# Startup of a fused attention and gated-dense kernel: task order, a second state buffer, moved neighbour sums and a moved weight copy

## The chip, the cores and the metric

The kernel runs on one core of a Trainium2 chip. The metric is the device time of one execution in microseconds (us), and the number compared is the median of several runs. Five parts of the core matter: TensorE (PE) with its weight loads (PEld), VectorE (DVE), ScalarE (ACT), GpSimd (POOL), and SyncE (SP), which issues all DMAs here. Each has its own queue of instructions and works through it strictly in order; they meet only through semaphores.

## The reference

Three computations follow each other: a linear attention with a decaying state, a gated dense part, and a mixture of four experts.

```python
def _attn_ref(q, k, v, alpha) -> np.ndarray:          # (4, 8, 768, 48) each
    state = np.zeros((B, H, D, D), dtype=np.float32)
    for t in range(S):
        state = alpha[:, :, t, :, None] * state + np.einsum('bhd,bhe->bhde', k[:, :, t], v[:, :, t])
        y[:, :, t] = np.einsum('bhd,bhde->bhe', q[:, :, t], state)

def _moe_ref(x, w_gate, w_val, w_out) -> np.ndarray:  # x: 3072 x 384, d_ff 1536
    gate = 1.0 / (1.0 + np.exp(-(x @ w_gate)))
    return (gate * (x @ w_val) @ w_out).astype(np.float32)

def _moe2_ref(x, domain_probs, w1, w2) -> np.ndarray: # 4 experts of 1024
    for e in range(E):
        out += p[:, e:e + 1] * (np.maximum(x @ w1[e], 0.0) @ w2[e])
```

## The kernel before

**Tiling.** The 768 positions of each of the 4 batches are cut into chunks of 128, so there are 24 attention *steps*, numbered 0 to 23 here. Three steps make one tile of 384 tokens for the gated dense part, which for each of 12 slices of d_ff runs a `gate` group, a `value` group (9 matmuls each into one bank) and an `out` group (9 matmuls). The experts come after all 8 tiles and are not touched here.

**One attention step.** The pairs inside a chunk are covered by six *levels* (`LVL`): at each, ACT spreads the needed columns of q into `QX` (L958), PE multiplies them with k (L695, L698), and the result goes into the matrix `AT`, by DVE under a mask for levels 0 to 2 (L1235) and by ACT for levels 3 to 5 (L929, L935). DVE multiplies k and q by the decays after each level (L1177); the next level's spread waits for that. Then come `TRK` (PE turns k, ACT copies it to `Kn`), `STATE` (PE makes the chunk's addition to the state from `Kn` and `V`, DVE scales the old state `ST` and adds it: L1249, L1255), `YOUT` (PE multiplies q with the state of the step before, L714, and `V` with `AT`, L718; DVE adds the part of the nearest neighbours and writes `ynat`, L1243) and `TRX` (PE turns `ynat`, ACT and DVE write its high and low half, `xT0h` and `xT0l`).

**Neighbour sums.** The terms of a position with itself and with the position before it are made apart: POOL multiplies rows (`near_products`, L1468 to L1471, three instructions), DVE sums them over each head (`near_sums`, L1204, into `near`), POOL multiplies with V and adds (`near_terms`, L1478 twice and L1484, into `y_near`). `near` and `y_near` have two buffers each.

**The first three steps.** They have no dense work to stand beside. They run in the order of the list `FIRST`, which all engines follow. The tasks use three banks of PSUM in turn, so that each task waits for the reader of the task three places before. At its end `first_part` does gate and value of slice 0 for the tokens of steps 0 and 1 (256 columns), and then for those of step 2 (128 columns). Then the tile loop starts: the remaining groups of tile 0, with the tasks of steps 3, 4 and 5 in slots between them. `prepare(0, 3)` on DVE (L1186, L1188, L1192) reads the k, q and decays of step 3, and stands in DVE's queue ahead of the first product of gate and value (`hid`, L1270).

**Weights.** `w_gate`, `w_val` and `w_out` arrive in three pieces each and are split into a high half, a rounded copy (`WGh` and so on), and a low half, the difference (`WGl` and so on). For the first three pieces `low_raw1(n)` does that on POOL: a cast (L1520) and a subtraction (L1522); of piece 0 alone the high half is made by ACT (`high_raw1(0)`, after level 2 of step 0). Piece 1 is the first of `w_val`, piece 2 the first of `w_out`. The semaphore `raw_split` counts the subtractions.

**The queue of SP.** There are six buffers for raw pieces, and piece n + 6 is loaded only when `raw_split` has reached n + 1. In the order of the queue:

```python
for n in range(len(pieces)):
    if n == len(pieces) - 1:
        load_step(0, STEPS_T)      # k, q and decays of step 3
        load_rows(0, STEPS_T)
    load_raw(n)                    # n >= 6 waits for raw_split >= n - 5
```

So piece 7 waits for the low half of piece 1, and what follows in the queue waits with it: first the `KQ` load of step 3 (which itself waits for step 1's state, y and neighbour terms), then `row` and `V` of step 3, then piece 8.

## Time and profile before

| | us |
|---|---|
| median of 3 runs | 1394.03 (1392.42 to 1394.73) |
| time of the profiled execution | 1391.0 |
| its span, first to last instruction | 1389.2 |
| PE busy | 1361.9 (98%) |
| POOL busy | 963.8 (69%) |
| DVE busy | 852.0 (61%) |
| ACT busy | 738.2 (53%) |
| TensorE clock granted | 1.0 over the whole span |

The page divides the span in 40 slices of about 35 us. PE is at nine tenths or more in nearly all of them; the first slice has 5 and the second 8 to 9. What is said below of the change concerns the first two slices. Times in the timeline are from the span's start; "x8" is a count of instructions merged into one row, and a bracket gives the idle time before and what ended it.

### The profile page before, as it was taken

How to read it: one execution, taken by the hardware profiler on the slowest of the kernel's cores; microseconds unless marked ns; L12 is line 12 of the kernel's file. 1: busy time of each engine (PE TensorE's matmuls, PEld its weight loads, DVE VectorE, ACT ScalarE, POOL GpSimd, SP SyncE). 2: the span in 40 equal slices, each digit the busy share in tenths (PEclk: the TensorE clock that was granted, in tenths of full speed). 3: DMA queues.
4: the chain of work that ended last, by engine and by line, in shares of the span. 5: the costliest groups of instructions: out<-in, count | busy, mean ns of one | idle time of the engine just before them, and what ended most of it. 6: DMA issues, size and time to landing. Idle time of an engine off the chain costs nothing.

```text
span 1389.2 us, 27651 instructions
## 1 busy us (share of the span) xinstructions
PE 1361.9 (98%) x10026; PEld 1261.6 (91%) x10026; DVE 852.0 (61%) x1335; ACT 738.2 (53%) x1467; POOL 963.8 (69%) x942
## 2 busy tenths in 40 slices
PE   5989999999999999999999999999999999999998
PEld 4989999999999999998999999999999999999998
DVE  7786555546464556343666666666766666666666
ACT  6664545445454455345555555555755555555552
POOL 6685545445445447477889898987897777777772
PEclk9999999999999999999999999999999999999999
DMA  9422221312121312002010101010121010101001
GB/s 326 122 76 89 89 75 55 109 56 84 62 75 55 109 55 88 13 1 69 24 46 24 46 24 45 23 46 23 46 92 46 24 46 24 45 23 45 23 12 68
DMA packets 42403, 83.37 MB, mean 60 GB/s; under 512 B 5824, under 2 KB 31168, under 8 KB 42304
## 3 DMA queue, kind: packets, MB, share of 16 engines
q1 hardware_dynamic: 42304, 82.01, 18.4%
q8 instruction: 67, 1.10, 0.3%
q14 instruction: 32, 0.26, 0.1%
HBM read 77.28 MB, written 4.72 MB: 59 GB/s over the span
## 4 chain that ended last, share of the span: by engine, by line
PE 95%; DVE 3%; ACT 1%; issue 1%; DMA 1%; POOL 0%; POOLq 0%; SPq 0%; ACTq 0%; DVEq 0%
PE PS L863 29%; PE PS L852 24%; PE PS L747 22%; PE PS L757 11%; PE PS L695 4%; PE PS L718 2%; PE PS L714 1%; PE PS L698 1%; DVE KQ L1177 1%; PE PS L703 1%; PE PS L726 1%; DMA KQ<-in_qka 1%; PE PS L731 0%; DVE AT L1235 0%; ACT QX L958 0%
## 5 line engine op out<-in xcount | busy, mean ns | idle before, releaser
L1417 DVE SCALAR_TENSOR_TENSOR acc<-PS,prob,acc 128x384 f32<-128x384 f32 x360 | 221.8, 616 | 209.6 <-PE PS L863 209.6
L958 ACT ACTIVATE QX<-KQ 48x256 f32<-48x256 f32 x288 | 120.8, 420 | 130.1 <-DVE KQ L1177 107.6
L1079 ACT ACTIVATE mixed<-PS 128x512 f32<-128x512 f32 x192 | 112.6, 589 | 89.8 <-PE PS L852 89.0
L1177 DVE TENSOR_TENSOR KQ<-KQ,TOT 112x512 f32<-112x512 f32 (+1 forms) x126 | 109.8, 894 | 43.6 <-PE PS L695 25.4
L1270 DVE TENSOR_TENSOR hid<-PS,hid 128x384 f32<-128x384 f32 x96 | 53.5, 558 | 128.2 <-PE PS L747 113.9
L1107 ACT ACTIVATE mixed<-mixed 128x512 f32<-128x512 f32 x192 | 118.4, 617 | 0.0
L1501 POOL TENSOR_TENSOR hs1l<-hid,hs1h 128x384 fp32r<-128x384 f32 x48 | 53.1, 1106 | 87.2 <-ACT hs1h L977 87.2
L1501 POOL TENSOR_TENSOR hs0l<-hid,hs0h 128x384 fp32r<-128x384 f32 x48 | 54.7, 1140 | 76.9 <-ACT hs0h L977 76.8
L695 PE MATMUL PS<-QX,KQ 112*64 112x64 f32 x1920 | 81.9, 237 | 20.4 <-ACT QX L958 19.7
L695 PEld LDWEIGHTS PS<-QX,KQ 112*64 112x64 f32 x1920 | 71.3, 148 | 32.8 <-issue 16.7
L1106 ACT ACTIVATE H_1h<-mixed 128x512 fp32r<-128x512 f32 x32 | 20.3, 634 | 129.9 <-DVE mixed L1391 129.9
L973 ACT ACTIVATE hid<-PS 128x384 f32<-128x384 f32 x96 | 47.2, 492 | 60.3 <-PE PS L747 57.4
L1461 POOL TENSOR_TENSOR TOT<-TOT 112x128 f32<-112x128 f32 (+2 forms) x126 | 43.2, 343 | 49.4 <-DVE TOT L1186 41.1
L1468 POOL TENSOR_TENSOR row<-row 128x384 f32<-128x384 f32 x24 | 24.2, 1007 | 63.7 <-DMA V<-in_v 63.7
L1235 DVE COPY_PREDICATED AT<-mask,PS 128x512 f32<-128x512 int32 x72 | 66.2, 919 | 0.5
L1629 POOL TENSOR_TENSOR H_0l<-mixed,H_0h 128x512 fp32r<-128x512 f32 x32 | 41.6, 1301 | 28.7 <-ACT mixed L1107 28.7
L1629 POOL TENSOR_TENSOR H_4l<-mixed,H_4h 128x512 fp32r<-128x512 f32 x32 | 41.5, 1297 | 24.5 <-ACT mixed L1107 24.5
L977 ACT ACTIVATE hs1h<-hid 128x384 fp32r<-128x384 f32 x48 | 25.2, 526 | 55.0 <-DVE hid L1270 55.0
L1629 POOL TENSOR_TENSOR H_5l<-mixed,H_5h 128x512 fp32r<-128x512 f32 x32 | 41.6, 1299 | 15.4 <-ACT mixed L1107 15.4
L1617 POOL TENSOR_TENSOR W_1l<-w_sum,W_1h 128x1408 fp32r<-128x1408 f32 x16 | 52.0, 3251 | 0.0
L1617 POOL TENSOR_TENSOR W_0l<-w_sum,W_0h 128x1408 fp32r<-128x1408 f32 x16 | 52.0, 3250 | 0.0
L747 PE MATMUL PS<-xT1h,WGh 128*128 128x384 f32 x144 | 50.1, 348 | 0.5 <-DVE xT1l L1263 0.5
(536 smaller groups left out, 4950.3 us busy)
## 6 DMA issues: line engine op xcount, KB each, us to landing
row<-in_rows SPq DMA_DIRECT2D x24, 768.0 KB, 4.4
KQ<-in_qka SPq DMA_DIRECT2D x24, 672.0 KB, 4.8
rawA<-in_w SPq DMA_DIRECT2D x32, 384.0 KB, 3.1
rawB<-in_w SPq DMA_DIRECT2D x32, 384.0 KB, 3.3
V<-in_v SPq DMA_DIRECT2D x24, 384.0 KB, 4.8
out_y<-acc SPq DMA_DIRECT2D x24, 192.0 KB, 2.2
raw<-in_w_gate SPq DMA_DIRECT2D x3, 768.0 KB, 13.9
raw<-in_w_val SPq DMA_DIRECT2D x3, 768.0 KB, 13.5
```

The source lines that it names most:

```text
L695: mm = pe.matmul(dst[mine, :, right], KQ[p][0:R, 1, a, mine], cols[:, :, right], start=True, stop=True)
L747: mm = pe.matmul(PS[:, bank, 0:T1], W[w][:, n, f * P:(f + 1) * P], xT[p][x][:, n, :], start=(n == 0 and (w, x) == SPLITS[0]), stop=(n == K ...
L757: mm = pe.matmul(PS[:, out_bank0 + n, 0:T1], WO[w][:, f, n * P:(n + 1) * P], hs[f % 2][x][:], start=(f == 0 and (w, x) == SPLITS[0]), stop ...
L852: mm = pe.matmul(PS[:, hidden_banks[HIDDEN[g]], :], W1[u % 2][w][:, WEIGHT[g], :], x_block(q, g)[x][:], start=n == 0 and g not in CONTINUE ...
L863: mm = pe.matmul(PS[:, result_banks[at % 4], 0:DM], h[x][:, t * P:(t + 1) * P], W2[u % 2][w][:, m, :], start=(m == 0 and (w, x) == SPLITS[ ...
L958: done = nc.scalar.activation(QX[p][rows, :, g, :].rearrange("d a (n t) -> d a n t", t=2 << level), right, ACT.Copy)
L1079: nc.scalar.activation(mixed[:, COPIED[g], :], PS[:, hidden_banks[HIDDEN[g]], :], ACT.Copy).then_inc(copied, 1)
L1107: nc.scalar.activation(mixed[:, part, :], mixed[:, part, :], ACT.Relu).then_inc(rh_ready, 1)
L1177: dve.tensor_tensor(x, x, y, ALU.mult).then_inc(kq_ready[p], 1)
L1417: dve.scalar_tensor_tensor(out=to, in0=result, scalar=weight, in1=to, op0=ALU.mult, op1=ALU.add).then_inc(acc_ready, 1)
L1501: nc.gpsimd.tensor_tensor(hs[f % 2][1][:], hid[f % 2][:], hs[f % 2][0][:].bitcast(F32), ALU.subtract).then_inc(hl_ready, 1)
L1629: nc.gpsimd.tensor_tensor(low[:], mixed[:, part, :], high[:].bitcast(F32), ALU.subtract).then_inc(rl_ready, 1)
```

## The change

- Order: in `FIRST`, `TRK` of step 1 comes ahead of `YOUT` of step 0, `STATE` of step 1 ahead of `YOUT` of step 1, and `YOUT` of step 2 between the `TRX` of steps 0 and 1. The gate part over steps 0 and 1 now follows `TRX` of step 2.
- State: a second buffer `ST1` holds the state after step 1. It lies over the last part of the low half of `w_val`, which is written much later.
- Neighbour sums: `near` gets a third buffer; the three `near_sums` on DVE move to after (level 5, step 0), (level 3, step 2) and (level 5, step 1). On POOL `near_products` of step 2 moves ahead of all `near_terms`, and `near_terms` of step 2 ahead of `low_raw1(1)`.
- Weight copy: the high half of piece 0 is made by POOL, and no more by ACT.

```diff
     if n == LEVELS:
-        FIRST += [(STATE, 0, 0), (YOUT, 0, 0), (TRK, 1, 0)]
-FIRST += [(YOUT, 1, 0), (STATE, 1, 0), (TRX, 0, 0), (TRX, 1, 0), (YOUT, 2, 0), (TRK, 2, 0), (TRX, 2, 0), (STATE, 2, 0)]
+        FIRST += [(STATE, 0, 0), (TRK, 1, 0), (YOUT, 0, 0)]
+FIRST += [(STATE, 1, 0), (YOUT, 1, 0), (TRX, 0, 0), (YOUT, 2, 0), (TRX, 1, 0), (TRK, 2, 0), (TRX, 2, 0), (STATE, 2, 0)]
...
+        ST1 = nc.alloc_sbuf_tensor_at("ST1", [P, PAIRS, 2 * D], F32, offset=top[0] - PAIRS * 2 * D * 4)
...
+        def state_of(i, sc):
+            return ST1 if is_first(i, sc) and sc == 1 else ST
...
-                if t == (YOUT, STEPS_T - 1, 0):
+                if t == (TRX, STEPS_T - 1, 0):
                     first_part("gate", 0, STEPS_T - 1)
-                if t == (TRX, STEPS_T - 1, 0):
                     first_part("value", 0, STEPS_T - 1)
...
-            high_after = {(LVL, 0, 2): 0}
...
-                if t in high_after:
-                    high_raw1(high_after[t])
...
-                        dve.tensor_tensor(ST[0:R], ST[0:R], tot_of(i, sc, C)[0:R].to_broadcast([R, PAIRS, 2 * D]),
+                        to = state_of(i, sc)
+                        dve.tensor_tensor(to[0:R], state_of(i, sc - 1)[0:R], tot_of(i, sc, C)[0:R].to_broadcast([R, PAIRS, 2 * D]),
...
-            sums_after = {(LVL, 0, 3): 0, (LVL, 0, 4): 1, (LVL, 1, 5): 2}
+            sums_after = {(LVL, 0, 5): 0, (LVL, 2, 3): 1, (LVL, 1, 5): 2}
...
-                if n == 0:
-                    pool.wait_ge(weight_high, 1)
-                else:
-                    pool.wait_ge(raw1_in[n], 16)
-                    nc.gpsimd.tensor_copy(high, raw_piece(n)).then_inc(own_high, 1)
-                    pool.wait_ge(own_high, n)
+                pool.wait_ge(raw1_in[n], 16)
+                nc.gpsimd.tensor_copy(high, raw_piece(n)).then_inc(own_high, 1)
+                pool.wait_ge(own_high, n + 1)
...
             low_raw1(0)
+            near_products(0, 2)
             near_terms(0, 0)
             near_terms(0, 1)
-            near_products(0, 2)
+            near_terms(0, 2)
             low_raw1(1)
-            near_terms(0, 2)
             low_raw1(2)
```

The queue of POOL between the row products of step 1 and the decays of step 3, before. `row_113` and `row_114` are the rows of steps 1 and 2, `raw_53` the raw pieces, `V_63`, `V_74`, `V_134` the V of steps 0, 1, 2:

```order
L1522 TENSOR_TENSOR WGl<-raw_53,WGh 128x3x512
L1478 TENSOR_TENSOR row<-V_63,near_81 128x384 x2
L1484 TENSOR_TENSOR y_near_83<-row 128x384
L1478 TENSOR_TENSOR row_113<-V_74,near_82 128x384 x2
L1484 TENSOR_TENSOR y_near_84<-row_113 128x384
L1468 TENSOR_TENSOR row_114<-row_114 128x384
L1469 TENSOR_TENSOR row_114<-row_114 128x384
L1471 TENSOR_TENSOR row_114<-row_114 128x384
L1520 CAST WVh<-raw_53 128x3x512
L1522 TENSOR_TENSOR WVl<-raw_53,WVh 128x3x512
L1478 TENSOR_TENSOR row_114<-V_134,near_81 128x384 x2
L1484 TENSOR_TENSOR y_near_83<-row_114 128x384
```

The same stretch in the changed kernel (its lines are 1 to 7 higher; `row_115`, `row_116`, `V_136` are now the names of steps 1 and 2, and `y_near_84` that of the first buffer):

```order
L1521 CAST WGh<-raw_53 128x3x512
L1523 TENSOR_TENSOR WGl<-raw_53,WGh 128x3x512
L1472 TENSOR_TENSOR row_116<-row_116 128x384
L1473 TENSOR_TENSOR row_116<-row_116 128x384
L1475 TENSOR_TENSOR row_116<-row_116 128x384
L1482 TENSOR_TENSOR row<-V_63,near_81 128x384 x2
L1488 TENSOR_TENSOR y_near_84<-row 128x384
L1482 TENSOR_TENSOR row_115<-V_74,near_82 128x384 x2
L1488 TENSOR_TENSOR y_near_85<-row_115 128x384
L1482 TENSOR_TENSOR row_116<-V_136,near_83 128x384 x2
L1488 TENSOR_TENSOR y_near_84<-row_116 128x384
L1521 CAST WVh<-raw_53 128x3x512
```

A cast is added at the head, and the split of piece 1 (`WVh`, `WVl`) now stands behind all three `y_near`, the last of which writes the buffer that step 0 used.

On PE, from the first `STATE` to the state matmuls of step 1, before (`AT_64` is step 0's, `KQ_65` step 1's, `KQ_125` step 2's):

```order
L726 MATMUL PS<-V_63,Kn 48x48 x8
L718 MATMUL PS<-V_63,AT_64 64x48 x16
L703 MATMUL PS<-ident,KQ_65 128x112 x4
L698 MATMUL PS<-QX_126,KQ_125 64x128 x4
L714 MATMUL PS<-ST,KQ_65 64x96 x2
```

and in the changed kernel (`KQ_127` is step 2's):

```order
L733 MATMUL PS<-V_63,Kn 48x48 x8
L710 MATMUL PS<-ident,KQ_65 128x112 x4
L725 MATMUL PS<-V_63,AT_64 64x48 x16
L705 MATMUL PS<-QX_128,KQ_127 64x128 x4
L733 MATMUL PS<-V_74,Kn 48x48 x8
L721 MATMUL PS<-ST,KQ_65 64x96 x2
```

The transpose of step 1's k moved up by one place and its `STATE` matmuls (`V_74,Kn`) moved ahead of its `YOUT`.

## Rows read from the trace of the kernel before

**Rows 1.** The page, the chain that ended last, by engine.

```profile
PE 95%; DVE 3%; ACT 1%; issue 1%; DMA 1%; POOL 0%; POOLq 0%; SPq 0%; ACTq 0%; DVEq 0%
```

**Rows 2.** Busy time by stretch: PE, PEld, DVE, ACT, POOL, then clock, DMA share, GB/s.

```profile
50.00:66.00 16.00, 16.00 (x135) 14.69 (x136) 12.43 (x18) 10.56 (x18) 9.19 (x12) 1.00 0.34 77
66.00:81.00 15.00, 12.59 (x123) 11.23 (x120) 15.00 (x17) 11.52 (x22) 11.59 (x14) 1.00 0.20 67
```

**Rows 3.** The chain of waits in order of time, two pieces of the start.

```profile
24.85 0.42 ACT QX L958
...
34.79 1.12 PE PS L695 x16
```

**Rows 4.** Timeline of ACT: start, duration, line, tiles.

```profile
18.73 1.49 ACT L1048 ACTIVATE WGh<-raw 128x1536 fp32r<-128x1536 f32 x1 [0.71 <-DMA raw<-in_w_gate]
20.12 1.69 ACT L958 ACTIVATE QX<-KQ 48x256 f32<-48x256 f32 x4
```

**Rows 5.** Timeline of DVE, from 21 to 52 us.

```profile
21.94 0.95 DVE L1204 TENSOR_REDUCE near<-row 128x16 f32<-128x768 f32 x1
22.80 0.69 DVE L1177 TENSOR_TENSOR KQ<-KQ,PS 112x512 f32<-112x512 f32 x1
...
38.37 0.56 DVE L1243 TENSOR_TENSOR ynat<-PS,y_near 128x384 f32<-128x384 f32 x1 [0.94 <-PE PS L718]
...
41.56 0.54 DVE L1249 TENSOR_TENSOR ST<-ST,PS 112x384 f32<-112x384 f32 x1
...
49.84 0.43 DVE L1186 TENSOR_TENSOR TOT<-KQ 112x256 f32<-112x256 f32 x1
...
51.44 0.56 DVE L1270 TENSOR_TENSOR hid<-PS,hid 128x384 f32<-128x384 f32 x1
```

**Rows 6.** Timeline of PE, from 36 to 53 us.

```profile
36.32 1.94 PE L718 MATMUL PS<-V,AT 128*64 128x48 f32 x32
38.19 0.60 PE L703 MATMUL PS<-ident,KQ 112*128 112x112 f32 x4
...
43.11 0.39 PE L714 MATMUL PS<-ST,KQ 112*64 112x96 f32 x4 [0.81 <-DVE ST L1255]
...
44.84 0.38 PE L780 MATMUL PS<-xT0h,WGh 128*128 128x256 f32 x1
...
52.09 0.40 PE L747 MATMUL PS<-xT0h,WVh 128*128 128x384 f32 x1
```

**Rows 7.** Timeline of POOL, from 18 to 41 us.

```profile
18.60 1.01 POOL L1471 TENSOR_TENSOR row<-row 128x384 f32<-128x384 f32 x1
...
29.89 1.00 POOL L1468 TENSOR_TENSOR row<-row 128x384 f32<-128x384 f32 x1
...
32.74 1.47 POOL L1520 CAST WVh<-raw 128x1536 fp32r<-128x1536 f32 x1
34.29 3.45 POOL L1522 TENSOR_TENSOR WVl<-raw,WVh 128x1536 fp32r<-128x1536 f32 x1
37.70 1.62 POOL L1478 TENSOR_TENSOR row<-V,near 128x384 f32<-128x384 f32 x2
39.40 1.00 POOL L1484 TENSOR_TENSOR y_near<-row 128x384 f32<-128x384 f32 x1
40.34 1.47 POOL L1520 CAST WOh<-raw 128x1536 fp32r<-128x1536 f32 x1
```

**Rows 8.** Timeline of SP: two issues.

```profile
37.77 0.37 SPq L612 DMA_DIRECT2D raw<-in_w_val  x1
41.41 0.33 SPq L592 DMA_DIRECT2D KQ<-in_qka  x1
```

**Rows 9.** SP's waits: who, for whom, total, times, longest.

```profile
SPq L612 <- POOL WVl L1522: 13.3, 1, 13.3
```

**Rows 10.** DMA issues by narrow window: KB, us to landing (issued 37.77, 41.41, 48.65).

```profile
raw<-in_w_val SPq DMA_DIRECT2D x1, 768.0 KB, 4.4
...
KQ<-in_qka SPq DMA_DIRECT2D x1, 672.0 KB, 4.6
...
KQ<-in_qka SPq DMA_DIRECT2D x1, 672.0 KB, 9.8
```

**Rows 11.** The first two KQ loads: waits of DVE, and the transfer's piece in the chain.

```profile
5.82 0.43 DVE L1186 TENSOR_TENSOR PS<-KQ 112x256 f32<-112x256 f32 x1 [1.66 <-DMA KQ<-in_qka]
...
8.41 0.43 DVE L1186 TENSOR_TENSOR PS<-KQ 112x256 f32<-112x256 f32 x1 [1.23 <-DMA KQ<-in_qka]
...
1.21 7.17 DMA KQ<-in_qka
```

More of the change, by code:

```diff
@@ L324, in attention_moe_program @@
         row = sb("row", [P, 4, DM])
-        near = [sb(f"near{p}", [P, 2, H]) for p in range(2)]
+        near = [sb(f"near{p}", [P, 2, H]) for p in range(3)]
         y_near = [sb(f"y_near{p}", [P, DM]) for p in range(2)]
@@ L507, in ynat_of, with near_of @@
             return ynat1 if is_first(i, sc) and sc == 1 else ynat
+        def near_of(i, sc):
+            return near[buffer_of(i, sc)]
+        def state_of(i, sc):
+            return ST1 if is_first(i, sc) and sc == 1 else ST
         def row_of(i, sc):
@@ L713, in task @@
                         for mine in sides if chunk else ():
-                            pe.matmul(bank[mine, a * 2 * D:(a + 1) * 2 * D], KQ[p][0:R, 0, a, mine], ST[0:R, a, :],
+                            pe.matmul(bank[mine, a * 2 * D:(a + 1) * 2 * D], KQ[p][0:R, 0, a, mine], state_of(i, sc - 1)[0:R, a, :],
                                       start=True, stop=False, skip_group_check=True)
@@ L1203, in near_sums @@
                 wait_apart(dve, products_ready, per_step(i, sc, 1, 1), sums_seen)
-                dve.tensor_reduce(near[sc % 2][:], row_of(i, sc)[:, 2:4, :].rearrange("p w (h d) -> p w h d", d=D), AX.X,
+                dve.tensor_reduce(near_of(i, sc)[:], row_of(i, sc)[:, 2:4, :].rearrange("p w (h d) -> p w h d", d=D), AX.X,
                                   ALU.add).then_inc(near_ready, 1)
@@ L1254, in task @@
                         if chunk:
-                            done = dve.tensor_tensor(ST[rows, :, mine], ST[rows, :, mine], new[rows, :, mine], ALU.add)
+                            done = dve.tensor_tensor(to[rows, :, mine], to[rows, :, mine], new[rows, :, mine], ALU.add)
                         else:
@@ L1283, in low_part1 @@
                 high, low = weight_parts(n)
-                dve.wait_ge(weight_high, n - 1)
+                dve.wait_ge(weight_high, n - 2)
                 done = dve.tensor_tensor(low[:, k], raw_piece(n)[:, k], high[:, k].bitcast(F32), ALU.subtract)
@@ L1479, in near_terms @@
                                             V[p][:, w].rearrange("p (h d) -> p h d", d=D),
-                                            near[sc % 2][:, w].unsqueeze(2).to_broadcast([P, H, D]), ALU.mult).then_inc(near_part, 1)
+                                            near_of(i, sc)[:, w].unsqueeze(2).to_broadcast([P, H, D]), ALU.mult).then_inc(near_part, 1)
                 pool.wait_ge(near_part, per_step(i, sc, 2, 2))
@@ L1526, in low_part1 @@
                 high, low = weight_parts(n)
-                pool.wait_ge(weight_high, n - 1)
+                pool.wait_ge(weight_high, n - 2)
                 done = nc.gpsimd.tensor_tensor(low[:, k], raw_piece(n)[:, k], high[:, k].bitcast(F32), ALU.subtract)
```

## Prediction

> **What bounds the kernel now.** I first read the page's chain of the work that ended last. PE is 95% of it [rows 1], so the kernel is a long row of PE work, and a change of the first 50 us counts only by how much earlier or later PE enters that row. The busy times by stretch show where it begins: PE is busy for all 16.00 us from 50 to 66, and from 66 to 81 for 12.59 of 15.00, while DVE is then busy for 15.00 [rows 2]. The work of that second stretch follows from the first (DVE's next product of gate and value waits for PE), so I treat what comes behind about 52 us as one rigid block, which moves with its first late piece. Next the chain of the start: from 24.85 it runs through ACT's copies without a gap to 34.79, where PE starts level 4 of step 2 [rows 3]; before 24.85 it is DVE. From 34.79 it alternates between PE and DVE, with one stall of PE, 0.81 us at 43.11, where step 2's YOUT waits for the state [rows 6].
>
> I take the start of the value group of slice 1, at 52.09, as the mark [rows 6]. It waits for the first `hid` of DVE, 51.44 + 0.56 = 52.00 [rows 5]. So PE's own queue and DVE's arrive within 0.1 us of each other: PE alone can gain nothing unless `hid` comes earlier too. This is the point on which I decide.
>
> **The change, part by part.**
>
> *Weight copy and neighbour sums.* ACT loses the copy of piece 0; from its start to the next one's is 20.12 - 18.73 = 1.39 us [rows 4]. DVE loses the first sum at 21.94, which costs 22.80 - 21.94 = 0.86 us there [rows 5], and the second, of the same form, a level later; both go to places where DVE waits for PE. The chain piece at 24.85 is an ACT copy that waits for DVE, so it comes earlier by the smaller of what both give: 0.86, not 1.39 + 0.86. ACT then runs through as before, and level 4 of step 2 starts at 34.79 - 0.86 = 33.93.
>
> *Order and second state.* From 33.93 I lay PE's tasks in the new order with their distances of before: the step 0 state matmuls at 34.8, step 1's k transpose at 35.46, step 0's YOUT at 35.98 (before 36.32), level 5 of step 2 after 1.87 us (38.19 - 36.32 [rows 6]) at 37.85. Then step 1's STATE 0.5 us on, its YOUT at 38.8. DVE's two steps for state 1 take 1.30 us (from 41.56 to 42.86, the point at which the stall ends [rows 5, 6]) and start about 1.5 us behind the level, at 39.3, so the state is there at 40.6. YOUT of step 2 follows at 40.75 without the stall, against 43.11: 2.4 us earlier. `ST1` costs no instruction; it only lets PE still read the old state while DVE writes the new. But gate now stands behind three transposes and needs step 1's x of both halves: TRX of step 1 at 42.5, ACT 0.5, DVE 0.6, each with its hand-over, which gives 44.2, against 44.84. Value follows at 45.4, and as nothing stands between the parts any more, PE's own arrival at the mark is near 50.9, a gain of 1.2 us. With the second sum and the third buffer of `near` nothing else moves: they only make the late sums possible.
>
> *POOL.* Here the bill comes. Its queue is free at 18.60 + 0.96 = 19.56. The added cast takes 1.55 and the subtraction 3.41 (34.29 - 32.74 and 37.70 - 34.29 [rows 7]): 24.5. The row products of step 2 take 2.85 (32.74 - 29.89): 27.4. Then POOL waits for the moved sums: the first ends at about 29.1, the second at 32.2. The terms take 1.70 + 0.94 each (39.40 - 37.70, 40.34 - 39.40 [rows 7]): 31.7, 34.9, and the products of the third end at 36.6. Its last addition writes the buffer that step 0's YOUT reads, so it waits for that: PE 35.98, plus the 2.05 from 36.32 to 38.37, plus 0.56 [rows 5, 6], makes 38.6. Only at 39.6 does the cast of piece 1 start, and its low half is there at 39.6 + 1.55 + 3.45 = 44.6, where it was 37.74. For the value part that is in time (45.4).
>
> *SP.* But SP holds piece 7 until then: it waited 13.3 us for this very subtraction before [rows 9] and issued at 37.77 [rows 8]. Now it issues at 44.6, and the KQ load of step 3, free at 41.41 before, is queued behind and goes at 45.0. Before it needed 4.6 us alone [rows 10] and landed at 46.0, 3.8 us before DVE took it up at 49.84 [rows 5]. That cover is gone.
>
> *When does it land?* No row shows a KQ load issued 0.4 us behind a full piece at this place. Lower bound: the piece ahead costs nothing, 45.0 + 4.6 = 49.6. Upper bound from rows of the same form: the KQ load with most in flight beside it took 9.8 [rows 10], 54.8. Nearest are the first two KQ loads, issued back to back in the same queue: DVE could start with them at 5.82 and 8.41, 2.6 us apart, and the second took 7.17 from its issue [rows 11]. Piece 7 took 4.4 from issue to landing [rows 10], so it lands at 49.0 and KQ 2.6 later at 51.6 (by the 7.17 it would be 52.2). I take 51.6. By the Trainium skill, DMA: Bandwidth & Descriptors, Anatomy of one DMA, a transfer costs about 2.0 us and its bytes at 436 GB/s; its fit is for another issuing path. For KQ alone (688 KB) that gives an estimate of 3.6 us, where the trace has 4.6, and for both loads in flight (1.47 MB) 5.4 us from 44.6, so 50.0 and 0.15 us over before at the mark.
>
> *DVE and the sum.* `prepare(0, 3)` stands ahead of `hid` in DVE's queue; from its start to the end of `hid` it is 52.00 - 49.84 = 2.16 us [rows 5]. With two hand-overs of 0.04: 51.6 + 2.24 = 53.84, later than PE's 50.9, so the gain of the front is lost, and the mark moves by 53.84 - 52.09 = +1.75 us. Behind it: POOL's decays of step 3 wait for the same KQ and end in time (before, the low half of `hid` had 0.5 us to spare, and both shift alike). Row and V of step 3 come later too; POOL needs them for the second low half, which had 1.3 us to spare. The KQ of step 4, issued at 48.65 before, is taken up only after 67 us. I cost these at nothing.
>
> Sum on the profiled execution: 1391.0 + 1.75 = 1392.8 (its span 1389.2 + 1.75 = 1390.9). That execution stood 3.0 us below the median of the runs, so for the median I predict 1394.03 + 1.75 = 1395.8 us.
>
> **The rivals.**
>
> *The load is not slowed by the piece ahead.* For it: SP issues them 0.4 us apart, and a lone load needed 4.6. Against it: the second of the first two loads landed 2.6 us behind the first. It lands at 49.6, the mark is at 51.84, and the time is 1394.03 - 0.25 = 1393.8: no change. (The estimate from the Trainium skill's page above, a landing at 50.0, belongs to this case too: 1394.2.)
>
> *The gain of the front arrives whole.* It needs `hid` by 50.9, so KQ by 48.7, less than 3.7 us after an issue at 45.0, or an issue by 44.1 at 4.6 us. For it: only if step 0's y, and with it POOL's split, comes a good microsecond earlier than I laid it. Time 1394.03 - 1.2 = 1392.8.
>
> *The load falls into a crowd (the slower side).* Row and V of step 3 are issued right behind KQ, and piece 7 ahead of it. If the four share the transfer engines instead of going one after the other, KQ needs as long as the 9.8 us that one took [rows 10]; say 9, landing at 54.0, and the mark is at 56.24, +4.15, 1398.2. It counts as slower from a landing at 52.65 on, which is +2.8. Against it: at 41.41 the same row and V were behind the KQ load, and it took 4.6.
>
> *The change does not do what it says.* If the moved sums made the late term of step 1 late for its YOUT, PE would stall near 40.7. `y_near` of step 1 is ready at 34.9 by my sum, 5.8 us before; I give it no chance of its own.
>
> **How the numbers follow.** The forecast (KQ from 50.5 to 52.6, so +0.7 to +2.8) gets 0.57; no slowing 0.18; the whole gain 0.07; the crowd 0.18. The own range of the forecast is 1394.7 to 1396.8. For 8 in 10, I leave out the end of the whole gain and the outer half of the crowd: 1393.1 to 1398.2. A measurement of this kernel tells about 0.2%, 2.8 us, from no change (its runs before lie 2.3 us apart). Forecast, no slowing and whole gain all lie inside it; the crowd lies outside. Faster 0.03, for what I have not seen and the spread of the medians; same 0.77; slower 0.20.
>
> **What would show it.** On ACT no weight copy near 18.7 and the copy at 24.85 near 24.0. On PE level 4 of step 2 near 33.9, YOUT of step 2 near 40.8 without a stall, the first gate part near 44.2. On POOL the subtraction of `WVl` ending near 44.6; on SP piece 7 right behind it and KQ at 45.0. On DVE an idle time ahead of `prepare(0, 3)` that a DMA of KQ ends, at 51.6, and a stall of PE ahead of the value group of slice 1, released by `hid` at 53.8. I am wrong if DVE does not wait there, or if PE idles elsewhere before 66 us, or if the stretch from 66 to 81 takes another length than before.

## The result, and the profile after

The changed kernel takes 1399.24 us, the median of 7 runs (1397.98 to 1401.02); the kernel before, run beside it, 1394.03 (7 runs). The ratio is 1.0035, with a 95% interval of 1.0024 to 1.0046: 5.2 us slower, where 1.75 were forecast. The time is 3.4 us above the forecast and 1.0 above the upper end of its range. The profiled execution took 1398.29 us, its span is 1396.4.

The chain that ended last, by engine, is nearly the one of [rows 1]:

```profile
PE 94%; DVE 3%; DMA 1%; issue 1%; ACT 1%; POOL 1%; POOLq 0%; SPq 0%; DVEq 0%; ACTq 0%
```

What is new in it stands in one place. This is the chain in order of time (start, duration, what), the answer to [rows 3]:

```profile
35.40 1.12 PE PS L702 x16
...
38.10 1.90 PE PS L725 x32
...
40.10 0.57 DVE ynat L1246
...
40.81 1.00 POOL y_near L1488
41.81 1.42 POOL WVh L1521
...
43.30 3.48 POOL WVl L1523
...
46.80 0.37 SPq L619
...
47.29 7.17 DMA KQ<-in_qka
...
54.48 0.43 DVE TOT L1189
...
56.08 0.57 DVE hid L1274
...
56.69 1.86 PE PS L754 x9
```

The chain runs from PE (step 0's YOUT, 38.10) to DVE, which writes `ynat`; to POOL, whose last neighbour sum may then reuse its buffer and whose split of piece 1 follows; to SP, which had waited for this split; to step 3's KQ load, to DVE's `prepare(0, 3)` and to the mark. Every link is one that the prediction named. Before, the two issues stood at 37.77 and 41.41 [rows 8], and DVE found KQ there at 49.84 [rows 5]. SP's wait for the split, 13.3 us in [rows 9], is now 19.9:

```profile
SPq L619 <- POOL WVl L1523: 19.9, 1, 19.9
```

On PE (start, duration, line; in brackets the idle time before and what ended it), the answer to [rows 6]:

```profile
43.66 0.39 PE L721 MATMUL PS<-ST,KQ 112*64 112x96 f32 x4
...
47.21 0.35 PE L787 MATMUL PS<-xT0h,WGh 128*128 128x256 f32 x1 [0.37 <-DVE xT0l L1267]
...
56.69 0.45 PE L754 MATMUL PS<-xT0h,WVh 128*128 128x384 f32 x1 [2.80 <-DVE hid L1274]
...
99.03 0.69 PE L702 MATMUL PS<-QX,KQ 112*64 112x64 f32 x16 [1.56 <-ACT QX L964]
```

The stall of 0.81 us ahead of step 2's YOUT is gone, as planned, and one of 2.80 us has come at the mark. By stretch (PE, PEld, DVE, ACT, POOL, then clock, DMA share, GB/s), the answer to [rows 2]:

```profile
50.00:66.00 16.00, 13.20 (x107) 12.23 (x104) 10.66 (x16) 7.98 (x14) 9.53 (x12) 1.00 0.79 226
66.00:81.00 15.00, 13.59 (x129) 12.00 (x127) 13.54 (x17) 11.53 (x23) 9.80 (x12) 1.00 0.01 2
...
99.00:104.00 5.00, 4.97 (x32) 4.93 (x33) 2.75 (x4) 3.43 (x8) 4.17 (x6) 0.66 0.00 0
```

PE lost 2.80 us between 50 and 66. The last row was not in the prediction at all: from 99.71, for 3.4 us, the granted clock is 0.50, the lower of TensorE's two levels (1.2 GHz), right behind PE's idle 1.56 us. The profile before has the same idle time, 1.54 us, at that place of the work and no such stretch.

**Where the 7.2 us between the two profiled spans lie.** DVE could start with the second KQ load at 8.41 before [rows 11] and at 9.80 after: 1.39 us of the start that has nothing to do with the change (in two further profiles of the changed kernel it is 8.42 and 9.02, in a second one of the kernel before 9.62). I therefore count the mark from that moment: 52.09 - 8.41 = 43.7 before, 56.69 - 9.80 = 46.9 after, so +3.2. From the mark to the end it is 1337.1 and 1339.7, so +2.6: about 1.5 lie where the clock is low, 1.1 spread over the experts. The fifteen profiles of this study without such a stretch, of whatever kernel, end 1336.6 to 1339.2 behind their mark, so that last 1.1 need not be the change's.

### The profile page after: what moved, and what is told of

The parts are those of the page before. It is cut to its first block, busy times and chain, and to the rows that moved or that the text cites. A ratio compares the mean times of both kernels' runs of the same rounds, so it can differ in the third digit from the quotient of the medians.

```text
span 1396.4 us, 27651 instructions
## 1 busy us (share of the span) xinstructions
PE 1366.4 (98%) x10026; PEld 1268.3 (91%) x10026; DVE 854.8 (61%) x1335; ACT 737.5 (53%) x1466; POOL 966.7 (69%) x943
## 4 chain that ended last, share of the span: by engine, by line
PE 94%; DVE 3%; DMA 1%; issue 1%; ACT 1%; POOL 1%; POOLq 0%; SPq 0%; DVEq 0%; ACTq 0%
PE PS L869 29%; PE PS L858 24%; PE PS L754 22%; PE PS L764 11%; PE PS L702 4%; PE PS L725 1%; DMA KQ<-in_qka 1%; PE PS L721 1%; PE PS L705 1%; DVE KQ L1180 1%; PE PS L710 1%; PE PS L733 0%; PE PS L738 0%; DVE AT L1238 0%; ACT QX L964 0%
## 5 line engine op out<-in xcount | busy, mean ns | idle before, releaser
L1465 POOL TENSOR_TENSOR TOT<-TOT 112x128 f32<-112x128 f32 (+2 forms) x126 | 43.2, 343 | 47.9 <-DVE TOT L1189 39.7
L754 PE MATMUL PS<-xT0h,WVh 128*128 128x384 f32 x141 | 49.7, 352 | 2.8 <-DVE hid L1274 2.8
```

The lines of the kernel that those rows point to most:

```text
L754: mm = pe.matmul(PS[:, bank, 0:T1], W[w][:, n, f * P:(f + 1) * P], xT[p][x][:, n, :], start=(n == 0 and (w, x) == SPLITS[0]), stop=(n == K ...
```

## The experiments

The first table has the place of the mark in each kernel's profile, counted from the second KQ load, and the executions with a low stretch. For each execution the mean granted clock is known to three digits. It is 1.000 or, where the record begins with some 17 us at half clock ahead of 41 us, 0.994; those executions are not longer (mean span 1391.6 in either case in the kernel before). Any other value (0.999, 0.998, 0.993, 0.991 and so on) means that the clock fell once the work was running.

| kernel | median us | ratio to before (95%) | mark behind KQ | clock fell |
|---|---|---|---|---|
| before (two profiles) | 1392.9 to 1394.2 | 1 | 43.7, 44.4 | 29 of 128 |
| changed (three profiles) | 1399.24, 1400.43, 1399.28 | 1.0035, 1.0052, 1.0036 | 46.9, 47.7, 48.3 | 17 of 17 |
| e2 KQ load ahead of piece 7 | 1393.24 | 0.9999 (0.9990 to 1.0008) | 44.0 | 2 of 11 |
| e3 split ahead of the sums | 1392.69 | 0.9992 (0.9983 to 1.0001) | 44.0 | 3 of 11 |
| e4 before, third buffer | 1394.8 | 1.0009 (0.9999 to 1.0019) | 44.1 | 3 of 11 |
| e5 before, KQ load late | 1395.31 | 1.0011 (1.0002 to 1.0020) | 46.0 | 7 of 11 |
| e6 order and state only | 1393.09 | 0.9989 (0.9980 to 0.9998) | 45.0 | 1 of 11 |
| e7 front only | 1392.66 | 0.9995 (0.9986 to 1.0004) | 42.9 | 0 of 11 |
| e8 copy only (one execution) | 1394.4 | | 43.9 | 0 of 1 |
| e9, e18 before, split late | 1395.22, 1395.92 | 1.0011 (1.0000 to 1.0021), 1.0013 (1.0004 to 1.0023) | 46.9, 46.0 | 11 of 21 |
| e10 both repairs | 1391.99 | 0.9987 (0.9978 to 0.9996) | 43.0 | 0 of 11 |
| e11 KQ load very late | 1403.24 | 1.0079 (1.0061 to 1.0098) | 51.2 | 4 of 4 |
| e12 front, KQ load first | 1392.7 | 0.9997 (0.9988 to 1.0007) | 42.6 | 3 of 11 |
| e13 idle time filled | 1397.84 | 1.0038 (1.0023 to 1.0053) | 48.5 | 2 of 7 |
| e14, e15 filled from 16 us on | 1399.24, 1393.41 | 1.0052, 1.0006 (0.9996 to 1.0015) | 49.2, 44.7 | 0 of 15 |

**The changed kernel again (e1).**

> The changed kernel once more, to see which parts of its trace belong to it. Queue theory (the late low half of piece 1 holds the KQ load of step 3 on SP): again DVE idle about 3 us ahead of prepare(0, 3), ended by the KQ load, and PE idle 2.8 us ahead of the value group of slice 1; time 1397.5 to 1401. Start theory (the first two KQ loads are slower in this kernel): the second lands at 9.8 again, where before it was 8.4. If the start is chance, it lands anywhere from 8.3 to 10, here and in the others. Clock theory: TensorE's granted clock falls to half near 100 us again; if that is chance too, it does not.

Measured 1400.43 us. The KQ load of step 3 took 8.2 us here; PE's wait at the mark (who, for whom, total, times, longest):

```profile
PE PS L754 <- DVE hid L1274: 4.5, 1, 4.5
```

The second KQ load came at 8.42 this time, so the late start of the first profile was chance, while the wait was longer.

**The KQ load ahead of piece 7 (e2), the split ahead of the neighbour sums (e3).** Each takes one link out of the chain above.

```diff
-                if n == len(pieces) - 1:      # e2
+                if n == len(pieces) - 2:
                     load_step(0, STEPS_T)
...
+            low_raw1(1)                       # e3
             near_terms(0, 2)
-            low_raw1(1)
```

> The changed kernel with one edit on SP: the KQ, row and V loads of step 3 stand ahead of piece 7 in the queue. Queue theory: KQ is issued at about 43.3 (step 1's y is done), lands by 48, DVE does not wait for it, and the 3.0 us between PE's own arrival (53.7) and the value group of slice 1 (56.7) go: 1399.2 - 3.0 = 1396.2. By PE's own queue it still gains nothing on before. Rival (the loss comes from the start, the clock or the addresses): 1399 as the changed kernel. Rival of my prediction (the gain of the front arrives whole once KQ is early): 1394.0 - 1.2 = 1392.8.

> The changed kernel with one edit on POOL: the split of piece 1 stands ahead of the neighbour terms of step 2, as before the change. Queue theory: the low half is ready at about 41.8, not 46.8, piece 7 goes then and KQ at about 43.3; the neighbour terms of step 2 are ready at about 44.4, 1.2 us ahead of their use. So as the SP edit: about 1396.2, and DVE does not wait for KQ. Rival (POOL's new work makes the neighbour terms late instead): step 2's y waits for POOL, and 1 to 2 us of the loss stay.

Either alone takes the whole loss away. I had expected 1396.2 us of both, the 3.0 us of PE's wait taken from the loss; both came out some 3 us lower still, the first sign that the wait costs more than its length. SP in e2 (start, duration): KQ no longer waits for the split, piece 7 goes as late as before the edit.

```profile
42.05 0.33 SPq L599 DMA_DIRECT2D KQ<-in_qka  x1
...
46.26 0.38 SPq L619 DMA_DIRECT2D raw<-in_w_val  x1
```

POOL in e3: the subtraction ends at 41.16 instead of 46.77, and KQ is issued at 42.78.

```profile
37.72 3.44 POOL L1523 TENSOR_TENSOR WVl<-raw,WVh 128x1536 fp32r<-128x1536 f32 x1
```

So the late load is necessary for the loss, and its way leads through POOL and SP.

**The third buffer's place (e4).** Only `near` gets a third, unused buffer in the kernel before.

```diff
-        near = [sb(f"near{p}", [P, 2, H]) for p in range(2)]
+        near = [sb(f"near{p}", [P, 2, H]) for p in range(3)]
```

> The kernel before with a third buffer of near that nothing uses: all later addresses move by 64 bytes, and no instruction. Queue theory: nothing depends on it, 1394.0, ratio 1.000. Address theory (the slower first loads and the slow drift of 1 us over the experts come from moved addresses): 1 to 2.5 us more, and the drift is in the trace.

No difference that can be told (1.0009, interval down to 0.9999), and its end lies 1337.4 us behind the mark, as before. An effect of the addresses on the loss of 5 us is excluded; one of 1 to 2 us is not.

**A late load without the rest (e5).** The kernel before with KQ, row and V of step 3 behind piece 8.

```diff
+                load_raw(n)
                 if n == len(pieces) - 1:
                     load_step(0, STEPS_T)
                     load_rows(0, STEPS_T)
-                load_raw(n)
```

> The kernel before with one edit on SP: the KQ, row and V loads of step 3 stand behind piece 8 instead of ahead of it, so KQ goes at about 45.8 instead of 41.4. Nothing else of the change is in it. Queue theory: KQ lands 7 to 8 us later, at 53 to 54, DVE and then PE idle for about 3 us before the value group of slice 1. Clock theory (an idle of PE of 3 us here is followed by a stretch at half clock, within some 50 us): that stretch is in the trace, 3.4 to 7 us long, and costs half its length. Both together: 1394 + 3.2 + 1.7 to 3.4 = 1399 to 1400.6, as the changed kernel. Rival (the fall of the clock belongs to the new order of the tasks, not to the idle): 1397.2, and no half clock after the start.

DVE waits for KQ (start 52.31, idle 1.92 us before), and the mark is 2.4 us later than in the first profile of before:

```profile
52.31 0.43 DVE L1186 TENSOR_TENSOR TOT<-KQ 112x256 f32<-112x256 f32 x1 [1.92 <-DMA KQ<-in_qka]
```

The time, 1395.31, is well below the 1399 to 1400.6 that I had expected. The load took 6.2 us instead of 7 to 8, so PE's wait was 1.7 us instead of 3, and the clock fell in 7 of 11 executions and not in this profile.

**The change cut in two (e6, e7), and the copy alone (e8).** e6 has the new order, `ST1` and the later first parts, and keeps ACT's copy and the neighbour sums and POOL's queue of before. e7 has the copy on POOL, the third buffer and the moved sums, with piece 1 split ahead of the near additions and the order of before. e8 has the copy alone (the counts that other waits compare with are lowered by one to match):

```diff
-            high_after = {(LVL, 0, 2): 0}
+            high_after = {}
...
-                if n == 0:
-                    pool.wait_ge(weight_high, 1)
...
+                pool.wait_ge(raw1_in[n], 16)
+                nc.gpsimd.tensor_copy(high, raw_piece(n)).then_inc(own_high, 1)
```

> The new order of the tasks, the second state buffer and the later first parts alone; sums, weight copy and POOL's queue as before. By the SP edit's trace the front's 0.8 us were there and the mark (value group of slice 1, counted from the landing of the second KQ load) was 0.26 later than before, so the order alone should cost about 1.0 at the mark, because its tasks fall in the stretch before TensorE's clock rises and gate waits for step 1's x. Theory: 1395, KQ issued at 41 to 42, no wait of DVE for it. Prediction's step (order gains 0.3 to 0.4 at PE's own arrival): 1393.6. Rival (the order is what costs 5 us): 1399.

> The weight copy on POOL, the later sums with their third buffer, and step 2's row products early, but with the old order, one state, and the split of piece 1 ahead of the neighbour terms of step 2. Theory: level 4 of step 2 starts 0.8 earlier (26.4 - 0.8 after the second KQ load's landing, which was 34.79 - 8.38 before), PE keeps its old order and all of it arrives: the mark 0.8 earlier, 1393.2. Rival (nothing of it arrives, because DVE or the KQ load is late next): 1394.0.

> Only the weight copy of piece 0 on POOL; all else as before. One look at the trace, as the size is below what the timing tells. Theory (the chain comes earlier by the smaller of what ACT and DVE give): DVE still does the first sum where it was, so level 4 of step 2 gains 0 to 0.1, not 1.39. POOL's cast comes on top: near terms 1 us later, not late for any use. Rival (ACT was the bound): level 4 of step 2 starts 1 us or more earlier.

Neither half loses anything (0.9989, 0.9995), so neither the order nor the front is at fault. The marks say more: 42.9 in e7 against 44.0 (the mean of the four profiles with the order and the sums of before: two of before, e4, e8), so the front gains 1.1 us; 45.0 in e6, so the order loses 1.0. The copy alone gains nothing (43.9): level 4 of step 2 starts 26.38 us behind the second KQ load in e8, as in the kernel before, and 25.6 behind it in every profile in which the sums have moved too. So DVE's sum was what the chain waited for, as the prediction had it. Why the order loses can be read on DVE, in e6 and then in e7, where step 2's state update releases `prepare(0, 3)` and `hid` behind it:

```profile
51.07 0.55 DVE L1256 TENSOR_TENSOR ST<-ST,PS 112x384 f32<-112x384 f32 x1 [2.19 <-PE PS L733]
```

```profile
48.89 0.56 DVE L1254 TENSOR_TENSOR ST<-ST,PS 112x384 f32<-112x384 f32 x1 [0.32 <-PE PS L733]
```

From the second KQ load (9.71 and 9.59) these are 41.4 and 39.3. In the new order gate and value over steps 0 and 1 stand behind all three transposes and directly ahead of step 2's state matmuls, so DVE waits 2.19 us for them, then still has 2.9 us of its own until `hid` starts. That the time of e6 is below that of before, though its mark is later, stays unexplained. Its profile was of the slowest of its executions (1394.75), so 45.0 may be late; by the times no cost of the order can be told. That the order costs some 0.9 at the mark rests on the marks of e2, e3 and e10 (43.0 to 44.0) beside those of e7 and e12 (42.6 and 42.9).

**The one line alone (e9).** The kernel before, in which the split of piece 1 alone moves.

```diff
-            low_raw1(1)
             near_terms(0, 2)
+            low_raw1(1)
```

> The kernel before with one edit: on POOL the split of weight piece 1 stands behind step 2's last near addition instead of ahead of it (as in the changed kernel; everything else, the order of PE too, as before). Theory (this one line is what makes the KQ load late): the addition can't start before step 0's y is read at 38.4 + 0.6; in the changed kernel the split ended 6.7 us after that read began (40.10 to 46.77), so here at 45.1; piece 7 issued at 45.1, step 3's KQ at 45.6, landed with the 7.17 of the changed kernel's profile at 52.8, value group of slice 1 at 55.0 instead of 52.1 (46.6 behind the landing of the second KQ load, where before has 43.7): +2.9 us, about 1396.7, with TensorE idle some 3 us ahead of it. Rival (the order of PE is needed too, or the loss is in the two states): no more than 0.7 us, 1393.8 to 1394.5.

The mark is where it is in the changed kernel, 46.9, by the same wait:

```profile
54.43 0.43 DVE L1186 TENSOR_TENSOR TOT<-KQ 112x256 f32<-112x256 f32 x1 [2.78 <-DMA KQ<-in_qka]
```

But the time is only 1.0011 of before, 1395.22 where I had expected 1396.7. That profile was of the slowest execution of this kernel (1397.8 us), and the clock fell in it; a second profile stands at e18.

**Both repairs (e10), the load later still (e11), the front alone with the load first (e12).** e10 is the changed kernel with the edits of e2 and e3; e11 the changed kernel with the edit of e5; e12 is e7 with the edit of e2.

> The changed kernel with both repairs: step 3's KQ, row and V loads ahead of weight piece 7 on SP, and the split of piece 1 ahead of step 2's near additions on POOL. Theory (either repair alone already takes the whole wait away, 1393.2 and 1392.7): nothing is added by the second, 1392.2 to 1393.5. Rival (piece 7, late in the one with the KQ load first, still costs): 1391.5 or less.

> The changed kernel with step 3's KQ, row and V loads behind weight piece 8 as well, so that KQ is issued at about 52.3 instead of 47.3 and lands at 57 to 59.5. Theory (the KQ landing sets the value group of slice 1, and a long idle stretch of TensorE is followed by one of granted clock 0.50): value group at 59.2 to 61.7 (56.7 in the changed kernel's profile), +2.5 to +5 us, and a clock stretch of 0.50 behind it that costs another 0 to 2 us over the one of the changed kernel: 1402 to 1406. Rival (the falls of the clock in the two profiles of the changed kernel were chance): no stretch of 0.50 between 45 and 110 us, 1400 to 1402.

> The kernel before with the cheap parts of the change only (copy of piece 0 on POOL, three near buffers and the sums in their new places, split of piece 1 ahead of the near additions, the old order of PE and one state) and step 3's KQ, row and V loads ahead of weight piece 7. Theory (KQ was waited for by nobody in that kernel, 1392.66): the same as without the new place of the loads, 1392.2 to 1393.2. Rival (the KQ load, no longer behind a weight piece, lands sooner and lets DVE prepare step 3 sooner, on the chain): 1391.5 to 1392.1.

e10 has the lowest median of the study, 1391.99 us, a ratio of 0.9987 with an interval that ends at 0.9996, so it is about 2 us faster than before; against e6, e3 or e7 the difference is inside the noise. e11 moves the mark by 4.3 us against the changed kernel's first profile (3.5 against the mean of three) and the median, of 4 executions, by 4.0. e12 is no better than e7: where the split is not late, the load's place in SP's queue is worth nothing to the time. It shows what the piece ahead costs the load, though: issued 0.49 us behind piece 7 in e7, KQ took 7.2 us, and ahead of it in e12 4.2; row and V of step 3 followed 2.2 to 3.0 us behind in both. DVE in e11:

```profile
58.58 0.43 DVE L1189 TENSOR_TENSOR TOT<-KQ 112x256 f32<-112x256 f32 x1 [7.71 <-DMA KQ<-in_qka]
```

**Filling the idle time (e13).**

```diff
+                    if isinstance(i, int) and i + tc == 0 and (kind, f) == ("value", 1):
+                        for _ in range(16):
+                            pe.matmul(PS[:, out_bank0 + 1, 0:T1], WG[0][:, 0, 0:P], xT[0][0][:, 0, :], start=True, stop=True)
                     group(i, tc + nxt, kind, f)
```

> The changed kernel, plus 16 matmuls of 384 columns on PE right ahead of the value group of slice 1 (into a bank that nobody reads before it is overwritten), in the place where PE idles 2.8 to 4.5 us: 16 x 0.17 = about 2.7 us of work that the result doesn't need. Theory (the late KQ load costs twice: the wait itself, and a stretch of granted clock 0.50 that follows the idle PE and costs about 2 us): with the idle time filled the value group starts where it did (about 56.7 to 57), but most executions show no stretch of 0.50 after 45 us (12 of 12 of the changed kernel had one, 13 of 81 of the kernel before); the median falls from about 1399.2 to 1400 to 1396.5 to 1397.5. Rival (the stretches of 0.50 are a sign of something else, or cost nothing): as many of them, or 1399 to 1400.5.

The load took 9.0 us this time, so the mark was later (57.64) and PE still idled 2.59 us behind the 2.94 us of filling:

```profile
52.12 2.94 PE L778 MATMUL PS<-xT0h,WGh 128*128 128x384 f32 x16
57.64 0.45 PE L754 MATMUL PS<-xT0h,WVh 128*128 128x384 f32 x1 [2.59 <-DVE hid L1277]
```

The clock around the mark, in e9 and in e13 (window, busy times, then clock, DMA share, GB/s):

```profile
57.00:61.00 4.00, 4.00 (x28) 3.45 (x27) 0.99 (x2) 1.73 (x4) 3.71 (x6) 0.57 0.86 151
```

```profile
57.00:65.00 8.00, 7.36 (x65) 6.73 (x66) 5.88 (x7) 5.83 (x10) 6.79 (x10) 1.00 0.59 115
```

In e13 the clock fell in 2 of 7 executions, against 17 of 17 of the changed kernel. So PE's idle time brings the low stretch about in most executions. Its length alone does not decide: this profile has a wait of 2.59 us and no fall, that of e9 one of 2.54 and a fall. What it costs can be read within one kernel: the mean span is 1393.3 with a fall and 1391.6 without in the kernel before (29 and 99 executions), 1395.0 and 1392.4 in that of e9 and e18 (11 and 10): 1.7 and 2.6 us. In the second pair a slow KQ load may bring both a later mark and the fall, so 2.6 may hold some of the mark. Free of it is the way from the mark to the end of the span: 1339.4 to 1341.4 in the five profiles with a low stretch (the three of the changed kernel, e9, e11), 1336.6 to 1339.2 in the fifteen without; the means, 1340.0 and 1337.8, are 2.2 apart. The gain of e13 in the median was below what I had expected (1397.84 us, but the kernel before was at 1392.88 beside it): its interval overlaps those of the changed kernel, so the time alone would not show it.

**Filling the start (e14, e15).** Both repairs, and one or two fp32 matmuls of 128 columns behind each level from step 0's level 2 on.

```diff
+                    if is_first(i, sc) and (j, level) not in ((0, 0), (0, 1), (1, 0)):
+                        if (j, level) == (0, 2):
+                            pe.wait_ge(*rows_landed(0, 0))
+                        for _ in range(1):                       # e15: range(2)
+                            pe.matmul(PS[:, out_bank0 + 1, 0:P], V[0][:, 0, 0:P], V[0][:, 0, 0:P], start=True, stop=True)
```

> The changed kernel with both repairs, plus one fp32 matmul of 128 columns behind each level from step 0's level 2 on, in the gaps in which PE waits for ACT (0.5 to 1.8 us each), to see whether a fuller PE gets the granted clock up before 38 us; a matmul row of a level then takes 0.69 instead of 1.12 us. Theory (what PE does there decides when the clock rises): rise earlier than 34 us, and 1 to 4 us gained, 1388 to 1391. Rival (the rise comes at its own time, or the added work delays the levels): rise at 38 to 42 as before, 1391.5 to 1394.

> As the one with one matmul behind each level, but two of them: PE is then busy for nearly all of 20 to 35 us. Theory: rise of the clock earlier still, 1388 to 1391. Rival: each added pair costs the level behind it 0.2 to 0.4 us, 1393 to 1397.

Against e10 (0.9987) one matmul costs 9 us (1.0052), two cost 2.6 (1.0006). PE at the same levels, in e14 and then in e15:

```profile
28.01 1.12 PE L702 MATMUL PS<-QX,KQ 112*64 112x64 f32 x16
29.06 0.80 PE L711 MATMUL PS<-V 128*128 128x128 f32 x2
```

```profile
28.32 0.69 PE L702 MATMUL PS<-QX,KQ 112*64 112x64 f32 x16
28.94 0.71 PE L711 MATMUL PS<-V 128*128 128x128 f32 x4
```

In e15 the clock record says full speed from 22.49 on, in e14 only from 44.26, and in all other profiles from 37.8 to 42.5. At full clock a level takes 0.69 us instead of 1.12, but its filling another 0.57 (28.32 to 28.94 to the next level at 29.58, a step of 1.26), so nothing is left of it. In e14 the step is 1.78 at the low clock, and levels that had waited for ACT now wait for PE. The theory was right on the clock in e15 alone, and its price was wrong in both: 1388 to 1391 us was expected, and e14's 1399.24 lies above its rival's range too.

**Second profiles (e16, e17, e18)** of the kernel before, the changed kernel, and that of e9.

> The kernel before once more, unchanged, for a second profile. Its first profile was of an execution 3.0 us faster than the median. Theory (what a profile shows of the mark is typical, only the start varies): value group of slice 1 at 43.7 to 44.1 behind the second KQ load, no wait for step 3's KQ. Rival (that profile was luck, and in a typical execution the mark is later by a microsecond or two, so that a late KQ costs less than the profiles show): 45 or more, or a wait of DVE for step 3's KQ.

> The changed kernel once more, unchanged. Theory: KQ issued 37.3 to 37.5 behind the second KQ load, landing 7 to 9 us later, mark at 46.9 to 48.5, a stretch of granted clock 0.50 after 45 us in every execution; ratio 1.0035 to 1.0052. Rival (the two profiles so far and the falls were chance): a mark at 46 or less, or executions without such a stretch.

> The kernel before with the split of piece 1 behind step 2's last near addition, once more. Its profile had the mark of the changed kernel (46.9 behind the second KQ load), but its time was only 1.0011 of before, against 1.0035 and 1.0052. Theory (that profile was its slowest execution, 1397.8 us, and a typical one loads KQ faster): mark at 45 to 46. Rival (the mark is the same, and the changed kernel loses its other 2 to 3 us elsewhere): mark at 46.7 to 47.5 in an execution of some 1395 us.

DVE's start with step 3 in e16, e17 and e18, in this order:

```profile
51.81 0.43 DVE L1186 TENSOR_TENSOR TOT<-KQ 112x256 f32<-112x256 f32 x1
```

```profile
55.13 0.43 DVE L1189 TENSOR_TENSOR TOT<-KQ 112x256 f32<-112x256 f32 x1 [5.22 <-DMA KQ<-in_qka]
```

```profile
52.41 0.43 DVE L1186 TENSOR_TENSOR TOT<-KQ 112x256 f32<-112x256 f32 x1 [1.52 <-DMA KQ<-in_qka]
```

The first profile of before was a little early (43.7, now 44.4, where I had expected 44.1 at most), the first of the changed kernel too (46.9, then 47.7 and 48.3), that of e9 late (46.9, now 46.0). KQ is issued at the same moment in all profiles of the latter two kernels, 37.3 to 37.5 behind the second KQ load. Only its time in flight differs: 7.2, 8.2 and 8.6 us in the changed kernel, 7.2 and 6.4 in the other.

## Why the prediction was wrong

The path that the prediction named, from step 0's YOUT over POOL, SP and KQ to the mark, held link by link. What failed are two sizes of the sum, the landing of KQ (6.6 us from its issue laid, 7.2 to 8.6 measured) and, smaller, POOL's split (0.8 later than laid), and one assumption, that everything behind the mark is a rigid block: behind the mark the changed kernel loses another 2 us or so to a stretch of low clock.

- *The front.* Level 4 of step 2 was to come 0.86 earlier. From the second KQ load it starts at 26.38 before and 25.60 after: 0.78. ACT's copy is gone, the sum of 21.94 is gone from DVE. Right.
- *The order.* The stall at 43.11 is gone, but "PE's own arrival at the mark is near 50.9, a gain of 1.2 us" was wrong. I laid gate at 44.2; it comes at 47.21, by the second KQ load 37.4 where I had 35.8. YOUT of step 0 alone is 0.66 later than I laid it, since the transpose in front of it takes 0.94 us and not the 0.5 that I allowed; YOUT of step 1 is 1.1 later and that of step 2 1.5. PE's own arrival at the mark (the mark less PE's idle time) is 43.2 to 44.1 behind the second KQ load in the three profiles, where I laid 42.5. I also looked at PE's queue only: DVE's state update of step 2 waits for matmuls that now stand behind both first parts. With the wait for KQ removed the mark is at 43.0 to 44.0 (e10, e2, e3), so the order eats the gain of the front. In the forecast this did not matter, because KQ came later than either.
- *POOL and SP.* `WVl` was laid to end at 44.6, or 36.2 behind the second KQ load; it ended 37.0 behind. The 0.8 are YOUT's delay of 0.66 and small change. KQ was issued 37.5 behind, for 36.6 laid.
- *The landing*, the term that was mis-sized most. The range of the forecast ended at a landing 7.6 us behind KQ's issue. I took 2.6 us behind a piece that takes 4.4, so 6.6 from KQ's issue (7.17 was the other value named). Piece 7 itself took 5.0, 6.7 and 6.9 and KQ 7.2, 8.2 and 8.6. The rival "crowd" put 9 there; the first profile is nearer to my 6.6, the other two are nearer to the rival. The traces bear its picture out: from 49 to 55 us of the first profile the DMA share is 1.03 at 343 GB/s, and row and V, issued right behind KQ, took 8.6 and 9.2, so all four were in flight together. The piece ahead is shown to slow KQ (7.2 in e7, 4.2 in e12). What row and V add is not: with row 0.4 us behind KQ and no piece ahead it took 4.6 and 5.0 in the kernel before. The two rows of KQ (KB, us from issue to landing) in the first profile and in e1:

```profile
KQ<-in_qka SPq DMA_DIRECT2D x1, 672.0 KB, 7.2
```

```profile
KQ<-in_qka SPq DMA_DIRECT2D x1, 672.0 KB, 8.2
```

  The estimate that the prediction works out from the Trainium skill, DMA: Bandwidth & Descriptors, Anatomy of one DMA, a landing 5.0 us after KQ's issue, is too low for this place by 2.2 to 3.6 us.
- *DVE from KQ to the mark*: 2.24 laid, 2.21 measured (54.48 to 56.69). Right.
- *One rigid block behind the mark.* Wrong. In all 17 executions the clock fell, which it did in 29 of 128 before, and the fall has a price of its own, 1.7 to 2.6 us. The term stood at nothing in the sum.

The sum over executions: the mean span is 1397.94 after (17 executions) and 1391.98 before (128), 5.96 apart. The mark moved from 44.0 (the mean of the two profiles of before, and of e4 and e8, which order this stretch alike) to 47.6 (three profiles): +3.6. The forecast's +1.75, with 0.8 for POOL and 0.6 to 2.0 for the landing, gives 3.2 to 4.6, which are the 3.2 to 4.6 of the three profiles against the first one of before. The low clock adds 1.7 to 2.6 us in all executions instead of 23% of them, so 1.3 to 2.0. Together 4.9 to 5.6; the remaining 0.4 to 1.1 us stays open. For e9 and e18 the same sum gives 2.4 for the mark and 0.5 to 0.8 for the clock, 2.9 to 3.2, and the mean span is 1393.79, +1.8; for e5 it gives 2.0 and 0.7 to 1.1, and the mean span is 1.7 above before. From one or two profiles a kernel, a mark is known to no better than a microsecond. So the late load is shown to be necessary for the loss (e2, e3), but the one line that makes it late brings only 1.8 of the 6.0 us by itself (e9, e18). A faster landing in its typical executions would account for that; it is not shown.

It is also open whether the load really is slower in the changed kernel (7.2 to 8.6 us in three profiles) than in the one of e9 (6.4 and 7.2 in two), and why, though both issue it at the same moment behind the same piece.

## What to carry to other kernels

When work is moved behind a wait on one engine, look for the semaphore that another queue waits on, and at everything behind that wait: here one subtraction of 3.4 us held back a weight piece that nobody was in need of, and behind it a load that somebody was. A load that is moved to a place behind another one needs room for the slowest landing seen in such a place, not for the one that looks nearest. And a new wait of 2 to 5 us on TensorE is not charged once: look at the granted clock behind it, in several executions, before taking the rest of the kernel as a block that only shifts.

## What the runs showed of the hardware

- TensorE's granted clock fell to the lower level after an idle stretch, though not at a fixed distance. In e1 and e17 (PE idle 4.5 and 5.0 us) it fell at 55.22 and 56.14, in e9 (2.5 us) at 57.27, in e11 (7.5 us) at 57.71, so in three of them while PE still waited (marks 56.16, 57.34, 60.79) and in e9 0.6 us behind its mark; in the first profile of the changed kernel (2.8 us) only at 99.71, behind a second idle time of 1.56 us; the same idle time, 1.54 and 1.51 us, stands in both profiles of the kernel before without a fall. The stretches lasted 3.4 or 6.8 us. The profiles of e5 (1.7 us), e18 (1.3) and e13 (2.6) have none. The Trainium skill, TensorE: Matmul & The Clock Gate, HAM oscillation, warns that waits of PE for DMAs send its clock back to the lower level. The runs agree: with PE's wait the clock fell in 17 of 17 executions, with 2.9 us of it filled in 2 of 7.
- In the profile with two added matmuls a level the clock rose at 22.49, where it rises at 37.8 to 42.5 us without any. In the profile with one, in which PE is also busy for the whole stretch, it rose at 44.26. The stretch from 23 to 38, in e14 and then in e15:

```profile
23.00:38.00 15.00, 15.00 (x144) 12.01 (x142) 9.86 (x23) 10.69 (x30) 7.96 (x7) 1.00 0.78 282
```

```profile
23.00:38.00 15.00, 13.95 (x209) 11.59 (x208) 12.47 (x29) 13.90 (x39) 10.82 (x11) 1.00 0.75 270
```

  Both say 1.00, but e14's matmuls take 1.12 us a level there: where the record of the clock begins late, the view fills what is missing with 1.00, and only the matmuls' durations tell the level. So it is with the 1.0 over the whole span in the table of the kernel before: its record begins at 38.22, and the level at 34.79 takes 1.12 us where that at 94.39 takes 0.69.
- The same KQ load of step 3, 672 KB, took 4.6 and 5.0 us in the kernel before and 4.2 to 6.0 in the others where no piece was issued within a microsecond ahead of it (save e3: 6.9, at 1.6 us behind a piece), and 6.2 to 9.0 us (9.0 in e13) issued 0.5 us behind a piece of 768 KB.
